# A fused attention and mixing kernel: query and token rows in nine tiles instead of ten

## What is computed

```
q_p, k_p = phi(q), phi(k)                 # phi: outer product of two 8-wide sketches, 64 features
kv  = einsum('bhsf,bhsd->bhfd', k_p, v);  z = sum(k_p, axis=2)
x   = (q_p @ kv) / (q_p @ z + 1e-6)       # then heads side by side: [4, 1088, 128]
...
mixed = real(fft(fft(x, axis=1), axis=2));  u = x + mixed
un = (u - mean(u)) / sqrt(var(u) + 1e-6)
x2 = u + relu(un @ w_ch1) @ w_ch2         # 128 -> 512 -> 128
...
h = relu(x2 @ w_in)                       # 128 -> 1024
conv_out = 3-tap convolution of h along the tokens
out = (h * sigmoid(conv_out)) @ w_out     # 1024 -> 128
```

## Time and profile before

| | us |
|---|---|
| median of 3 runs | 286.53 (286.39 to 286.85) |
| the profiled execution, its own time | 254.52 |
| its span | 252.7 |
| PE busy | 244.1 |
| PEld busy | 215.2 |
| DVE busy | 219.6 |
| ACT busy | 167.9 |
| POOL busy | 46.0 |

### The profile page before, as it was taken

How to read it: one execution, slowest core, us unless ns; L and a number is a source line. 1 busy time by engine, 2 the same in 40 slices (tenths; PEclk the granted TensorE clock), 3 DMA queues, 4 the chain that set the end, 5 groups by cost and what they waited for, 6 DMA issues and landing times.

```text
span 252.7 us, 4417 instructions
## 1 busy us (share of the span) xinstructions
PE 244.1 (97%) x1555; PEld 215.2 (85%) x1555; DVE 219.6 (87%) x404; ACT 167.9 (66%) x337; POOL 46.0 (18%) x114
## 2 busy tenths in 40 slices
PE   8999999999999999997999999999999999999975
PEld 6999999999989998996988788888998888977742
DVE  0757888899998697897979999999999989999992
ACT  2342634332576556778899688989777999968632
POOL 0000000000614541565401220130200231210000
PEclk9999999999999999999999999999999999999999
DMA  7968830210000020000004724637620498952002
GB/s 220 342 258 296 361 100 3 56 45 0 3 0 0 4 83 1 3 3 3 0 0 88 178 83 95 176 137 220 176 91 2 174 225 220 236 116 88 1 3 88
DMA packets 7798, 26.40 MB, mean 104 GB/s; under 512 B 1120, under 2 KB 1888, under 8 KB 7776
## 3 DMA queue, kind: packets, MB, share of 16 engines
q0 software_dynamic: 3456, 13.34, 20.8%
q1 hardware_dynamic: 4176, 12.74, 14.0%
q10 hardware_dynamic: 144, 0.03, 0.1%
HBM read 10.54 MB, written 2.23 MB: 51 GB/s over the span
## 4 chain that ended last, share of the span: by engine, by line
PE 50%; DVE 3%; ACT 2%; issue 1%; ACTq 0%
PE ps L696 14%; PE ps L605 10%; PE ps L606 10%; PE ps L607 10%; PE ps L645 5%; ACT arena L818 1%; PE ps L636 1%; DVE attic L1173 1%; DVE attic L1164 0%; DVE attic L1180 0%; ACT attic L904 0%; PE ps L615 0%; DVE x_room L1078 0%; DVE arena L1085 0%; DVE x2lo L1112 0%
## 5 line engine op out<-in xcount | busy, mean ns | idle before, releaser
L904 ACT ACTIVATE attic<-attic,base 128x1088 f32<-128x1088 f32 x32 | 37.9, 1209 | 11.9 <-DVE attic L1173 11.9
L696 PE MATMUL ps<-attic,wout 128*128 128x364 f32 (+1 forms) x126 | 40.9, 468 | 1.5 <-DVE attic L1180 1.5
L605 PE MATMUL ps<-x2hi,wlo 128*128 128x364 f32 x96 | 37.1, 386 | 0.8 <-ACT arena L832 0.4
L696 PEld LDWEIGHTS ps<-attic,wout 128*128 128x128 f32 x126 | 23.5, 189 | 14.6 <-DVE attic L1180 2.2
L607 PE MATMUL ps<-x2hi,whi 128*128 128x364 f32 x96 | 31.6, 329 | 0.0
L606 PE MATMUL ps<-x2lo,whi 128*128 128x364 f32 x96 | 31.5, 328 | 0.0
L605 PEld LDWEIGHTS ps<-x2hi,wlo 128*128 128x128 f32 x96 | 18.1, 188 | 5.0 <-ACT folded_room L889 1.2
L889 ACT ACTIVATE x_room<-ps 128x364 f32<-128x364 f32 x42 | 18.1, 478 | 3.9 <-PE ps L607 3.5
L606 PEld LDWEIGHTS ps<-x2lo,whi 128*128 128x128 f32 x96 | 18.1, 188 | 2.3 <-issue 1.1
L1173 DVE SCALAR_TENSOR_TENSOR attic<-x_room,ratio,attic 128x1088 f32<-128x1088 f32 x14 | 18.8, 1346 | 1.4 <-DMA attic<-x_room 1.3
L769 ACT ACTIVATE attic<-ps 109x320 f32<-109x320 f32 (+2 forms) x16 | 6.7, 425 | 18.9 <-PE ps L520 16.5
(11 more groups left out here) (127 smaller groups left out, 615.3 us busy)
## 6 DMA issues: line engine op xcount, KB each, us to landing
gate_hi<-attic POOLq DMA_DIRECT2D x11, 544.0 KB, 2.9
attic<-x_room POOLq DMA_DIRECT2D x7, 544.0 KB, 5.3
attic<-v_d SPq DMA_DIRECT2D x4, 594.0 KB, 4.0
attic<-qT_d SPq DMA_DIRECT2D x3, 545.0 KB, 6.6
attic<-kT_d SPq DMA_DIRECT2D x3, 544.5 KB, 5.7
attic<-folded_room POOLq DMA_DIRECT2D x3, 544.0 KB, 5.3
out_d<-arena SPq DMA_DIRECT2D x3, 544.0 KB, 4.0
attic<-arena POOLq DMA_DIRECT2D x2, 544.0 KB, 5.0
```

Of the source, the lines that this page charges most:

```text
L605: pe.matmul(out, lo, rhi, start=first, stop=False)
L696: pe.matmul(ps[:, OUT_BANK + t, 0:z - a], wout[:, c, :], gate(i)[:, a:z], start=(c == 0), stop=(c == C2 - 1)).then_inc(wout_done, 1)
L904: act.activation(gate(i), gate(i), ACT.Sigmoid, scale=base[:, i % C2:i % C2 + 1]).then_inc(gate_ready, 1)
```

## The change

The 545 tokens of the first half are cut otherwise: four tiles of 121 rows (`TQ`) and one rest of 61 tokens (`TM`, the middle). The four have mirror tiles of 121 rows as before. The middle and its mirror now share one tile of 128 rows (`WQ`): the 61 tokens in rows 0 to 60, their mirrors in rows 64 to 124, the others are zero. So there are nine query tiles instead of ten. In memory each query tile takes 128 columns of `qT`, and the attention stage treats all nine as 128 wide. The tables of cosines and sines get 128 columns too; those of the middle hold the mirrored outputs beside the direct ones, with the sign of the sine turned, so one sum makes both sides.

The ten units stay, with the same slots and tables. Eight hold four tiles of 121 rows, 484 columns. The two middle units (4 and 7, at places 4 and 9) hold two tiles of 128, 256 columns. `mirror_fold` becomes a copy of the mirrored 61 rows down to partition 0, two instructions on four tiles and two on the middle one, where one add and one subtract on five tiles stood before.

```diff
-TQ = HALF // NJ
-NQ = 2 * NJ
+TQ = 121
+TM = HALF - (NJ - 1) * TQ
+WQ = 128
+OTHER = 64
+NQ = 2 * (NJ - 1) + 1
...
+WIDE = [len(unit) for unit in UNITS]
+ROWS = [WQ if unit[0][2] == MIDDLE else TQ for unit in UNITS]
+COLUMNS = [rows * wide for rows, wide in zip(ROWS, WIDE)]
...
-AT_PIECES = [(0, 3), (3, 6), (6, 8), (8, 10)]
+AT_PIECES = [(0, 3), (3, 5), (5, 7), (7, NQ)]
...
-                    src, rows = (kT, TK) if side == 0 else (qT, TQ)
+                    src, rows = (kT, TK) if side == 0 else (qT, WQ)
...
-                for y in range(4):
-                    m = 4 * n + y
-                    mm = pe.transpose(ps[:, bank, y * TQ:(y + 1) * TQ],
+                for m in range(4 * n, min(4 * n + 4, 2 * NQ)):
+                    y = m - 4 * n
+                    mm = pe.transpose(ps[:, bank, y * WQ:(y + 1) * WQ],
...
-                for m in range(2 * BP):
-                    mm = pe.transpose(ps[:, bank, m * TQ:(m + 1) * TQ], un[:, r % 2, m, :], ident[0:TQ, 0:TQ])
+                for m in range(WIDE[unit]):
+                    mm = pe.transpose(ps[:, bank, m * rows:(m + 1) * rows], un[0:rows, r % 2, m, :], ident[0:rows, 0:rows])
...
-                three_pass(ps[:, bank_h1(n), 0:G1], whi[:, c * 128:(c + 1) * 128], wlo[:, c * 128:(c + 1) * 128],
+                three_pass(ps[:, bank_h1(n), 0:COLUMNS[r]], whi[:, c * 128:(c + 1) * 128], wlo[:, c * 128:(c + 1) * 128],
...
-                dve.tensor_tensor(fold[:], here, there, ALU.add).then_inc(fold_step, 1)
-                dve.tensor_tensor(odd[:], here, there, ALU.subtract).then_inc(fold_step, 1)
+                dve.tensor_copy(other, x_nat[OTHER:OTHER + TM, b, NQ - 1, :]).then_inc(fold_step, 1)
+                dve.tensor_tensor(fold[:, low], here, there, ALU.add).then_inc(fold_step, 1)
+                dve.tensor_tensor(odd[:, low], here, there, ALU.subtract).then_inc(fold_step, 1)
+                dve.wait_ge(fold_step, 6 * b + 1)
+                dve.tensor_tensor(fold[0:TM, MIDDLE], middle, other, ALU.add).then_inc(fold_step, 1)
+                dve.tensor_tensor(odd[0:TM, MIDDLE], middle, other, ALU.subtract).then_inc(fold_step, 1)
...
-                for side in range(2):
+                for side in range(mixes(r) // 2):
```

More of the change, by code:

```diff
@@ L431, in _ @@
             pool.memset(half[:], -0.5).then_inc(half_set, 1)
+            for tile in (fold, odd):
+                pool.memset(tile[:, MIDDLE, :], 0.0).then_inc(fold_zero, 1)
             for x2 in (x2hi, x2lo):
@@ L1014, in mirror_fold @@
             def mirror_fold(b):
-                here, there = x_nat[:, b, 0:NJ, :], x_nat[:, b, NJ:NQ, :]
+                low = slice(0, NJ - 1)
+                here, there = x_nat[0:TQ, b, 0:NJ - 1, :], x_nat[0:TQ, b, NJ - 1:2 * (NJ - 1), :]
+                middle = x_nat[0:TM, b, NQ - 1, :]
                 dve.wait_ge(x_ready, len(AT_PIECES) * (b + 1))
@@ L1089, in moments @@
                     dve.wait_ge(rstd_ready, r - 2)
-                for m in range(2 * BP):
-                    ins = dve.bn_aggr(mv[:, r % 3, m, :], stats[:, m, :])
+                for m in range(n):
+                    ins = dve.bn_aggr(mv[0:rows, r % 3, m, :], stats[0:rows, m, :])
                 ins.then_inc(mv_ready, 1)
@@ L1252 @@
     f = np.float32
-    pairs = np.concatenate([row_tokens(j) for j in range(NJ)])
-    assert sorted(pairs) == list(range(HALF))
-    order = np.concatenate([pairs, (S - pairs) % S])
+    assert sorted(np.concatenate([row_tokens(j) for j in range(NJ)])) == list(range(HALF))
     heads = [0, 1, 3, 2]
     channels = np.concatenate([np.arange(64), np.arange(127, 63, -1)])
-    qT = np.ascontiguousarray(q[:, heads][:, :, order].transpose(1, 3, 0, 2)).reshape(DM, B, NQ * TQ)
+    q_rows = q[:, heads].transpose(1, 3, 0, 2).reshape(DM, B, S)
+    qT = np.zeros((DM, B, NQ, WQ), f)
+    for j in range(NJ):
+        rows = row_tokens(j)
+        for side, tokens in enumerate((rows, (S - rows) % S)):
+            tile, first = (NQ - 1, side * OTHER) if j == MIDDLE else (side * (NJ - 1) + j, 0)
+            qT[:, :, tile, first:first + len(rows)] = q_rows[:, :, tokens]
+    qT = qT.reshape(DM, B, NQ * WQ)
     kT = np.zeros((DM, B, NK * TK), f)
@@ L1294 @@
                     values = np.where(out % 2 == parity, values, 0.0)
-                table[:TQ, TABLE_OF[j] + n, :] = values
+                table[:values.shape[0], TABLE_OF[j] + n, :values.shape[1]] = values
+                if j == MIDDLE:
+                    table[:values.shape[0], TABLE_OF[j] + n, OTHER:OTHER + TM] = values if part == 0 else -values
     cos_t, sin_t = cos_t.astype(f), sin_t.astype(f)
```

190 lines of the change are left out of this document (112 added, 78 removed).

## The result

The changed kernel takes 262.46 to 263.60 us where the kernel before takes 253.41 to 255.01: a ratio of 1.036, 95% interval 1.034 to 1.039, so it is slower by 3.6%. (All comparisons here are within the lower of two levels, some 33 us or more apart, into which the executions of every kernel fall; the 286.53 us given ahead is the upper level of the kernel before, and in the two traces taken in it, those of e2 and e9, all of the difference lies before the first token sum, which starts at 102.79 and 91.33 us there, while what follows runs as in the other traces.) The prediction had +1.5 us, 0.5%. The sign was right and the size was not: the profiled execution went from 254.52 to 262.46 us, its span from 252.7 to 260.6, +7.9.

What follows compares the result with a forecast made beforehand. PE was taken as the bound: its own work, then its few waits. Attention +0.6, slots 0 to 14 +2.0, waits -0.2, slots 15 to 22 -0.5, then down to +1.5: 286.53 to 288.0 us, range 285.5 to 289.5.

Steps and rivals of the forecast that it cites:

- Pitches: PE's start-to-start time per record, read from the earlier trace: 0.107 us for 128-column query products, 0.1095 for 128-column transposes.
- rival of dearer records: 128-column weight loads in the attention stage at 0.123 us a record: 291.4 us, or 289.7 at 0.115; chance 0.12.
- Attention stage, +0.6: Query sketches, products and transposes on nine 128-wide tiles take +0.14 us per batch, +0.6 over four.
- Slots 0 to 14, +2.0: Before slot 14's up ends, wider units' ups and downs add 1.8 us and longer transposes 0.2 to 0.3.
- the waits' -0.2: In slots 0 to 14, PE's two token-sum waits on DVE, some 0.15 us each, shrink: -0.2 us.
- Slots 15 to 22: PE's work falls 1.9 us, but DVE, POOL and ACT set the pace; by 118.43 only 0.5 us comes back.
- the chain's start: DVE's queue from its wait at 100.37 on, releasing POOL at 105.22, then ACT; place 7's release was put 0.87 us earlier against it.
- near 1.9 us in all (some of it before the down of slot 19): Sign to check: PE's wait for DVE before the transposes of place 7 grows to this from 0.98 us.
- first rival: In slots 15 to 22 PE's waits don't grow, sign a wait under 1.0 us at place 7: +0.6, 287.1 us; chance 0.25.
- After 118.43, -0.4: Later ups -0.1 us, downs about 0, unit 7's transposes -0.2; PE leaves the slots at +1.5 instead of +1.9.
- the relief wins: Faster, by query tiles at 0.096 us a record (285.0 us) or waits in 60 to 130 us all gone (285.4); chance 0.18.
- the waits don't grow: DVE, ACT and POOL reach slot 18 earlier, so PE's 0.9 us of longer waiting goes: +0.6, 287.1 us; chance 0.25.

Runs made afterwards that it cites:

- e2: The changed kernel with the middle tile held in 64 rows instead of 61 by adding zeros; ratio to the kernel before 1.0375.
- e9: The changed kernel with the middle tile padded to 121 rows, its last token sum in slot 19 instead of 18, mixed rows in slot 20; ratio 1.0173.
- e1: The padded kernel: the changed kernel with the middle tile held in 121 rows (added rows zero) in fold transposes, channel transform and token sums; ratio 1.0142, span 254.9 us.
- e4: The kernel before, with only the middle tile's term in the token sums on 61 rows instead of 109; ratio 1.0229.
- e5: The changed kernel with the channel stage's middle tile padded to 121 rows, its token-sum term still on 61; ratio 1.0312, span 259.3 us.
- e10: e1 with ups, downs and the copies between on 436 of a wide unit's 484 columns, the rest left out; ratio 1.0106, span 255.2 us.
- e7: The kernel before with units 4 and 7 worked on 256 columns instead of 436, the rest left out; ratio 0.997, span 251.6 us.
- e6: The changed kernel with the sine part's terms reversed, so the 61-row terms of a token sum stand adjacent; ratio 1.0287, span 259.7 us.

## Why the prediction failed, step by step

- **The omitted term.** The step that failed is the one on the token sums and the middle tile. The prediction saw that the middle tile's fold transpose is narrower ("fewer moving columns but the same weights") and left it at 0.095; it measured 0.20. It said nothing of the middle tile's term in the token sums, which went from 109 rows to 61 at an unchanged number of records. That term was costed at nothing, as if the 0.111 of the earlier trace rows held for any number of rows. The small operands cost 5.3 us of the 8.1 at the end (e1): up to slot 15, 4.7 and 4.9 in the sums (e4, e5), and 1.0 in the channel stage (e5). Without them the change costs 2.8 us (1.4%), where 1.5 was forecast. The Trainium skill ("TensorE: Matmul & The Clock Gate", LDWEIGHTS) says that the row count of a weight load doesn't matter and that one of 32 x 128 takes as long as one of 128 x 128. The loads' own times agree (179 ns with 61 rows and 183 with 121, L632), and so do the pitches among records of one size (0.11 for 61, 109 and 121 rows). What the price hangs on is the change from one size to the other, 0.20. No row of the trace of before could have bounded it, since it has no float32 matmul with 61 rows; the prediction should have said so.
- **Pitches.** A query product with 128 columns was forecast at 0.107; twelve records from 19.84 to 21.18 are 0.112, and the query sketches are 0.112 as well. The row that the 0.107 came from the earlier trace rows already had it: through a narrow window, its second record starts at 29.59, and the seven from there to 30.37 take 0.111 each. Only the first, behind a transpose, is shorter (0.08). So the pitch was mis-sized, and the prediction's own condition for its rival of dearer records, "from a pitch of 0.110 on", is met: 54 x 0.005 is 0.27 us more per batch, 1.1 over four. Transposes of 128, forecast 0.1095: four from 13.03 to 13.47, 0.11. Right.

```profile
29.59 0.94 PE L532 MATMUL ps<-attic 121*128 121x66 f32 x7
```

```profile
19.84 1.50 PE L595 MATMUL ps<-arena 128*128 128x66 f32 x12
21.18 0.58 PE L552 MATMUL ps<-sketch,attic 128*121 128x64 f32 x4
```

- **Attention stage, +0.6.** Counted from the first transposes to the first token sum, it is +0.70 in all padded kernels (45.44 against 44.74) and 1.00 in the changed one, whose small operands lie there too. The number is near the forecast, but by luck. In that stretch of the padded kernel, from start to start, the query products take 12.12 us instead of 11.56, the query sketches 4.01 instead of 3.83, the feature transposes 7.33 instead of 6.85; the key products, which the change doesn't touch, take 13.81 instead of 14.33, and that nobody forecast. Why they do isn't shown. The stretch also leaves out the sketches before it and the last batch's products behind it. The plain times of the first sum, 58.02 padded and 58.01 before, don't show the +0.70, since the start came 0.69 earlier.
- **Slots 0 to 14, +2.0.** 91.55 - 88.84 - 0.70 = 2.01 in the padded kernel. The sum is right to 0.2 (with the waits' -0.2 it was 1.8), its parts less so: 1.51 by columns instead of 1.8 (e10), and 0.50 for transposes and the rest instead of 0.2 to 0.3.
- **Slots 15 to 22.** Place 7 was forecast 0.87 earlier against the chain's start; in the padded kernel the difference falls from 2.71 to 1.84, by 0.87. Alone, in e7, it is 0.85. The wait forecast "near 1.9 us in all (some of it before the down of slot 19)" came as these two rows of the padded kernel:

```profile
114.94 0.36 PE L639 MATMUL ps<-h1hi,wlo 128*128 128x256 f32 x1 [0.66 <-DVE h1lo L1160]
...
116.44 0.60 PE L651 MATMUL ps<-ident,arena 121*128 121x121 f32 x4 [0.91 <-DVE late_lo L1152]
...
119.70 0.43 PE L639 MATMUL ps<-x2hi,wlo 128*128 128x364 f32 x1 [0.43 <-ACT arena L874]
```

  1.57 us. At the second hidden chunk 119.70 - 12.58 against 118.43 - 13.27 is +1.96, forecast +1.9. The sum hits from terms that are each some 0.3 off: it starts at 2.71 instead of 2.4, and loses 0.75 instead of 0.5. The chain itself was read rightly. In the changed kernel the waits are smaller (0.49 at place 7), since the slower sums had made PE late enough. By the prediction's own sign ("less than 1.0 there") this would have spoken for the first rival, wrongly.
- **After 118.43, -0.4.** Wrong: +0.8 in the padded kernel (2.78 at the end). The prediction let all of unit 7's relief count and had no new wait. There is one of 0.52 for ACT at 164.35 and one of 0.39 for DVE at 174.59, and e7 shows that 2.2 us of this relief are worth 0.9. The widths of units 8 and 9 count in full: from unit 8's down to unit 9's the padded kernel takes 18.68 and the kernel before 17.96.

```profile
164.35 0.44 PE L639 MATMUL ps<-x2hi,wlo 128*128 128x364 f32 x1 [0.52 <-ACT folded_room L931]
...
174.59 0.61 PE L672 MATMUL ps<-ident,x_room 121*128 121x121 f32 x4 [0.39 <-DVE x2lo L1166]
```

- **The rivals.** That the relief wins is out: 4.1 us of it give 0.9. That the waits don't grow is out, by the padded kernel (1.57 against 0.98). The rival of dearer records was right in part for the 128 columns (0.112, a third of the way to its 0.123), and it named the kind of cost that the small operands have, a pitch that falls back, but not their place. The range (to +3.0) didn't hold the result, as it was made of known shapes only.

## What to carry to other kernels

Cutting a tile to fewer rows saves TensorE nothing where the number of records stays, and can cost: when a float32 stream mixes operands of at most 64 rows or columns with larger ones, keep the small one above 64 with zeros, or put the small ones next to each other (e6 did, and kept 0.7 us of it at the end). In a forecast, list every operand shape that the change brings and that the trace of before doesn't hold, the small ones too. Relief on the engine that is busy longest counts only up to the next place where a chain of other engines is already the last to arrive: here two tenths of it.

## What the runs showed that I had not expected

- The pitch of float32 matmul records (130 moving columns, 109 to 128 stationary) is 0.11 us among operands of 61 rows, and for streams of 65, 96, 109 or 121 rows with 121 or 109; each change between 61 or 64 rows and 121 (or 109) makes two pitches of 0.20 to 0.22, the one up to the first record of the new size and the one behind it. 65 rows is as fast as 96. Operands of 128 rows and 61 columns do the same, at 0.16 to 0.21.
- A weight load's own busy time doesn't tell of it: with 121 columns it is 177 to 184 ns in both sizes. It shows in when the load starts (with its matmul and not 0.11 us ahead), in the pitches, and in the mean duration of the matmul records (320 against 274 ns).
- A copy of 544 KB by DMA with another transfer issued 0.54 us behind it landed in 2.9, 3.6 or 4.9 us at the same place of kernels that differ little, and the end moved by 1.0.
- Why the load isn't taken ahead at a change of size wasn't tested, nor whether it is so for other data types.
